# Mix matmuls cut into one piece per slot, with another order of work on VectorE and ScalarE

## The reference

```python
scores = scale * np.matmul(q, k.transpose(0, 1, 3, 2))
scores = scores + bias.transpose(2, 0, 1)[None, :, :, :]
scores = scores - np.max(scores, axis=-1, keepdims=True)
attn = np.exp(scores)
attn = attn / (np.sum(attn, axis=-1, keepdims=True) + 1e-09)
out = np.matmul(attn, v)
...
h = x @ w_in
x = (h * np.cos(h)) @ w_out
...
xn = x / rms * rms_g
g = xn @ w_gate
y = (silu(g) * (xn @ w_val)) @ w_out
```

## Time and profile before

| | |
|---|---|
| median of 3 runs | 1210.84 us |
| the profiled execution, its own time | 1210.84 us |
| its span, first to last instruction | 1209.1 us |
| busy: TensorE, weight loads | 97%, 89% |
| busy: VectorE, ScalarE, GpSimd | 58%, 41%, 40% |
| mean granted TensorE clock | 0.995 of full speed |

### The profile page before, as it was taken

How to read it: one execution, slowest core, us unless ns; L and a number is a source line. 1 busy time by engine, 2 the same in 40 slices (tenths; PEclk the granted TensorE clock), 3 DMA queues, 4 the chain that set the end, 5 groups by cost and what they waited for, 6 DMA issues and landing times. The chain is left out here.

```text
span 1209.1 us, 21829 instructions
## 1 busy us (share of the span) xinstructions
PE 1171.6 (97%) x7464; PEld 1081.3 (89%) x7464; DVE 702.2 (58%) x1540; ACT 494.7 (41%) x1034; POOL 483.8 (40%) x515
## 2 busy tenths in 40 slices
PE   5789999999989999999999999999999999999998
PEld 2268777778779999999999999999999999999998
DVE  8978888888889867777686887553011020110201
ACT  6967777777733433333343433111111111111111
POOL 3047777777776342525243353761111111111111
PEclk9989999999999999999999999999999999999999
DMA  5853525352234000000000011330000000000000
GB/s 173 248 180 119 168 93 176 100 181 75 67 108 128 19 2 1 0 0 0 0 0 0 0 35 35 105 114 27 1 1 26 0 26 0 0 26 0 26 0 26
DMA packets 46534, 69.06 MB, mean 57 GB/s; under 512 B 3712, under 2 KB 27424, under 8 KB 46496
## 3 DMA queue, kind: packets, MB, share of 16 engines
q1 hardware_dynamic: 46496, 68.60, 18.1%
HBM read 53.25 MB, written 15.34 MB: 57 GB/s over the span
## 5 line engine op out<-in xcount | busy, mean ns | idle before, releaser
L811 PE MATMUL banks<-x_high,w_low_rest 128*128 128x384 f32 x672 | 224.5, 334 | 0.0
L809 PE MATMUL banks<-x_high,w_high_rest 128*128 128x384 f32 x672 | 224.4, 334 | 0.0
L810 PE MATMUL banks<-x_low,w_high_rest 128*128 128x384 f32 x672 | 224.4, 334 | 0.0
L1358 DVE TENSOR_TENSOR X<-X,banks 128x384 f32<-128x384 f32 x72 | 39.8, 552 | 298.1 <-PE banks L811 298.0
L1377 POOL TENSOR_TENSOR product_low<-X,product_high 128x384 fp32r<-128x384 f32 x72 | 72.9, 1012 | 344.5 <-ACT product_high L1320 344.5
L1175 POOL TENSOR_TENSOR product_low<-g,product_high 128x384 fp32r<-128x384 f32 x96 | 102.6, 1069 | 236.6 <-ACT product_high L1057 236.6
L809 PE MATMUL bank<-product_high,w_high_rest 128*128 128x384 f32 x480 | 162.1, 338 | 0.8 <-POOL product_low L1175 0.8
L811 PE MATMUL bank<-product_high,w_low_rest 128*128 128x384 f32 x480 | 160.6, 335 | 0.0
L810 PE MATMUL bank<-product_low,w_high_rest 128*128 128x384 f32 x480 | 160.5, 334 | 0.0
L1085 ACT ACTIVATE angle<-angle,quarter 128x384 f32<-128x384 f32 x96 | 59.2, 617 | 202.1 <-DVE angle L1117 202.1
L588 ACT ACTIVATE probs<-probs,neg_max 128x576 f32<-128x576 f32 (+1 forms) x160 | 123.5, 772 | 18.4 <-DVE neg_max L638 18.1
(11 more groups left out here) (113 smaller groups left out, 2512.1 us busy)
## 6 DMA issues: line engine op xcount, KB each, us to landing
raw_qk<-in_qk SPq DMA_DIRECT2D x32, 576.0 KB, 3.8
bias_scratch<-bias_stage SPq DMA_DIRECT2D x36, 288.0 KB, 3.1
bias<-bias_scratch SPq DMA_DIRECT2D x32, 288.0 KB, 3.3
w_raw<-in_w_out SPq DMA_DIRECT2D x28, 256.0 KB, 2.6
values<-in_v SPq DMA_DIRECT2D x16, 320.0 KB, 4.0
w_raw<-in_w_in SPq DMA_DIRECT2D x16, 256.0 KB, 2.9
out_t<-X SPq DMA_DIRECT2D x5, 768.0 KB, 3.5
w_raw<-in_w_gate SPq DMA_DIRECT2D x12, 256.0 KB, 3.0
```

The source lines that it names most:

```text
L809: nc.tensor.matmul(out, high, x_high, start=start, stop=False)
L810: nc.tensor.matmul(out, high, x_low, start=False, stop=False)
L811: return nc.tensor.matmul(out, low, x_high, start=False, stop=stop)
```

## The change

- MIX_SLOTS is gone. `mix` takes a step c and does that step alone. Half 0 of pair n - 1 is done in slots 3 to 7 (c = 0 to 4), half 1 in slots 8 and 9 (c = 0, 1) and in slots 0 to 2 of the next pair (c = 2 to 4). Pieces c = 0 to 3 are two column matmuls; c = 4 is the full-width one. The waits stand at c = 0 and c = 4.
- EXP_LAG is 2 in place of 1: guard and invert treat the tile two slots back, normalise the one three back.
- On VectorE guard, normalise and invert stand ahead of add_bias; keep_mixed stands at the head of slot 3 (half 1) and slot 8 (half 0); keep_end comes in slot 4, in place of slot 3.
- On ScalarE the exponential of a slot stands ahead of the copy of the transposed tile.
- After pair 15 TensorE goes through ten slots without scores, so half 1's first two pieces come ahead of first_h and its other three behind it. The first of them waits for VectorE's copy of half 0.

```diff
--- before.py
+++ after.py
@@ -31,8 +31,7 @@
 TILES = 2 * NQ
 HS = S // 2
 QPAD = NQ * P
-EXP_LAG, T_LAG = 1, 4
-MIX_SLOTS = (4, 9)
+EXP_LAG, T_LAG = 2, 4
 EARLY_TILES = 3
 
 
@@ -533,22 +532,27 @@
                                                ident[0:rows, 0:rows])
                 last.then_inc(turned_ready, 1)
 
-            def mix(n, parity, half, first):
-
-                pe.wait_ge(att.values_in[parity], n * 8 + (16 - 8 * parity))
-                pe.wait_ge(copied, n * TILES + (NQ + 3) if half == 0 else (n + 1) * TILES)
-                if not (first and half == 0):
-                    pe.wait_ge(mixed_copied, n * 2 + half)
+            def mix(n, parity, half, c, first):
+
+                if c == 0:
+                    if half == 0:
+                        pe.wait_ge(att.values_in[parity], n * 8 + (16 - 8 * parity))
+
+                        pe.wait_ge(copied, n * TILES + (NQ + 3))
+                    else:
+                        pe.wait_ge(copied, (n + 1) * TILES)
+                        pe.wait_ge(last_end_copied, n + 1)
+                    if not (first and half == 0):
+                        pe.wait_ge(mixed_copied, n * 2 + half)
                 queries = slice(half * HS, (half + 1) * HS)
-                for c in range(NQ - 1):
+                if c < NQ - 1:
                     for h in range(2):
                         nc.tensor.matmul(mixed[h * D:(h + 1) * D, 0:HS], values[parity][:, c, h, :],
                                          probs_t[parity][:, h, c, queries], start=(c == 0), stop=False)
-                pe.wait_ge(end_copied, n + 1)
-                if half == 1:
-                    pe.wait_ge(last_end_copied, n + 1)
-                nc.tensor.matmul(mixed[:, 0:HS], values[parity][:, NQ - 1, :, :].rearrange("p h d -> p (h d)"),
-                                 probs_t_end[parity][:, queries], start=False, stop=True).then_inc(mixed_ready, 1)
+                else:
+                    pe.wait_ge(end_copied, n + 1)
+                    nc.tensor.matmul(mixed[:, 0:HS], values[parity][:, c, :, :].rearrange("p h d -> p (h d)"),
+                                     probs_t_end[parity][:, queries], start=False, stop=True).then_inc(mixed_ready, 1)
 
             def slot(n, parity, s, step, compute=True):
 
@@ -559,8 +563,12 @@
                         turn(n - 1, TILES - T_LAG + s, False)
                 elif compute:
                     turn(n, s - T_LAG, step == 0)
-                if step > 0 and s in MIX_SLOTS:
-                    mix(n - 1, 1 - parity, MIX_SLOTS.index(s), step == 1)
+                if s < 3:
+                    if step > 1:
+                        mix(n - 2, parity, 1, s + 2, False)
+                elif step > 0:
+                    half, c = divmod(s - 3, NQ)
+                    mix(n - 1, 1 - parity, half, c, step == 1)
 
             def pair(n, parity, step):
                 for s in range(TILES):
@@ -573,12 +581,13 @@
             with pe.Fori(1, PAIRS // 2) as m:
                 pair(m * 2, 0, 2)
                 pair(m * 2 + 1, 1, 2)
-            for s in range(MIX_SLOTS[0] + 1):
+            for s in range(TILES):
                 slot(PAIRS, 0, s, 2, compute=False)
 
             pe.wait_ge(biased, PAIRS * TILES)
             chunks.first_h(pe)
-            mix(LAST, 1, 1, False)
+            for c in range(2, NQ):
+                mix(LAST, 1, 1, c, False)
 
         @block.scalar
         def _(act):
@@ -605,11 +614,11 @@
 
             def pair(n, parity, first):
                 for s in range(TILES):
+                    exps(n, s)
                     if s >= T_LAG:
                         keep(n, parity, s - T_LAG)
                     elif not first:
                         keep(n - 1, 1 - parity, TILES - T_LAG + s)
-                    exps(n, s)
 
             pair(0, 0, True)
             pair(1, 1, False)
@@ -668,19 +677,21 @@
                     m, _, r = back(n, parity, s, EXP_LAG)
                     m3, _, r3 = back(n, parity, s, EXP_LAG + 1)
 
-                    if hp is not None:
-                        dve.wait_ge(att.bias_in[s], (hp + 1) * 16)
-                    add_bias(n, s, step == 0)
+                    if step > 1 and s == 3:
+                        keep_mixed(n - 2, 1)
+                    if step > 0 and s == 8:
+                        keep_mixed(n - 1, 0)
                     if s >= EXP_LAG or step > 0:
                         guard(m, r)
                     if (s >= EXP_LAG + 1 or step > 0) and r3 not in POOL_TILES:
                         normalise(dve, m3, r3, dve_normed)
                     if s >= EXP_LAG or step > 0:
                         invert(m, r)
-                    if step > 0 and s == T_LAG - 1:
+                    if hp is not None:
+                        dve.wait_ge(att.bias_in[s], (hp + 1) * 16)
+                    add_bias(n, s, step == 0)
+                    if step > 0 and s == 4:
                         keep_end(n - 1, 1 - parity)
-                    if step > 0 and s in MIX_SLOTS:
-                        keep_mixed(n - 1, MIX_SLOTS.index(s))
 
             pair(0, 0, 0, hp=0)
             pair(1, 1, 1)
@@ -699,6 +710,7 @@
                     normalise(dve, m3, r3, dve_normed)
                 if s < EXP_LAG:
                     invert(LAST, TILES - EXP_LAG + s)
+            keep_mixed(LAST - 1, 1)
             keep_end(LAST, 1)
             dve.wait_ge(mixed_copied, (LAST - B + 2) * 2)
             for k in DVE_PARTS:
```

## The result

The changed kernel takes 1233.3 us (median of 4 runs, 1232.49 to 1233.76), the kernel before 1210.62 us in the same comparison. The ratio is 1.0186, with a 95% interval of 1.0169 to 1.0204. The forecast was 1230, with a range of 1217 to 1240. The profiled spans are 1231.8 and 1209.1.

The account below looks back on a forecast made before the run. TensorE was taken as the bound, with about 16.0 us of work a pair. Steady pairs 15.1, pair 1 -0.7, pair 15 +3.0 and tail +1.5 sum to 18.9 on 1210.84: 1230 us, range 1217 to 1240.

Parts of the forecast that it names:

- VectorE's idle time: Steady pairs: VectorE idles 2.0 us a pair until the mix is done; better interleaving wins TensorE only 0.4 to 0.5.
- A change of form and back: TensorE going into the 64-wide form and out costs 0.34 us; a piece behind a 64-row transpose costs 0.64, not 0.83.
- The pair takes 17.66: Steady pairs 2 to 14: TensorE's work goes from 16.0 to 17.66 us, mix pieces costing 7.24 against 5.55; 15.1 in all.
- The new orders: VectorE's and ScalarE's work per pair lies under TensorE's 17.66 us, so VectorE's reordering and EXP_LAG 2 cost and win nothing.
- Part 4's tie: ScalarE's copy behind the exponential waits for its slot's addition; slot 3's transposes just covered, else up to 0.4 us, once or twice a pair.
- Pair 1 and pair 15: Pair 1 has fewer pieces and keeps 1.3 us of stalls: -0.7; the first nine slots of pair 15: +3.0.
- The tail: After pair 15, half 1's first piece waits for VectorE's copy ahead of first_h: +1.5 us, including 0.25 for a later split.

Follow-up runs that it names:

- kernel 4: Changed kernel with two-step column pieces in slots 0, 3, 5 and 8, the old tail, and ScalarE's copy ahead of its exponential: 1208.0 us.
- experiment 3: Changed kernel with each column piece as one full-width matmul in place of two of 64 columns, leaving out head 1's part of the mix: 1205.6 us.
- experiment 5: Changed kernel with EXP_LAG 1, VectorE's addition first and ScalarE's copy first, as in the kernel before: 1234.02 us.
- 6: Two-step kernel (kernel 4) with EXP_LAG 1 and VectorE's addition ahead of guard, normalise and invert: 1216.34 us.
- 9: As kernel 4, but each half's four column steps together in slot 3 or 8: 1225.66 us; also with EXP_LAG 1 and VectorE's addition first: 1238.85 us.
- experiment 7: Changed kernel with the mix in two whole blocks (slots 2, 7) and old tail: 1250.56 us; second, with ScalarE's copy ahead of its exponential: 1225.47 us.
- experiment 2: Changed kernel with 42 useless identity transposes on TensorE during the tail's wait for the copy of half 0: 1230.53 us.
- 8: Kernel before with its two whole mix blocks one slot earlier, in slots 3 and 8, and keep_end in VectorE's slot 2: 1218.72 us.
- experiment 1: Changed kernel with all five pieces of pair 15's half 1 behind first_h, as in the kernel before: 1228.53 us.

## Why the prediction was right, and where a term was off

- *TensorE is the bound, and VectorE's idle time is worth at most 0.5 a pair.* Right. VectorE's wait for the mix nearly went, and the pair grew from 16.49 to 17.70. The 0.5 was won in kernel 4, whose 16.33 are all work; its two more changes of form, which cost 0.3, leave 0.16 of it.
- *A change of form and back costs 0.34, 0.19 less behind a 64-row tile.* Right, and shown three ways: slots of 1.80, 1.90, 1.45 and 1.34 as worked out; 0.34 less per slot without the change (experiment 3); the pair at 16.33 with half the changes (experiment 4). The 0.19 is borne out by slot 8, which goes from 1.22 to 1.86, by 0.64, where slots 4 to 6 pay 0.83.
- *The pair takes 17.66.* 17.70. Over 13 pairs it is +15.7, for 15.1 forecast. The prediction's own terms (16.0 + 7.24 - 5.55) give 17.69; it wrote 17.66.
- *The new orders are hidden in the changed kernel.* Right (experiment 5). They stop being hidden when the pieces get fewer: VectorE's then wins 8 and 13 us (6 and 9), and ScalarE's costs 25 with whole blocks (7). ScalarE's order was not run with two-step pieces.
- *Part 4's tie just fits.* Right as far as it goes: no transposes wait for ScalarE in the steady pairs. Experiment 7 shows what it costs where it does not fit.
- *Pair 1 and pair 15:* -0.7 and +3.1, for -0.7 and +3.0. In pair 1 there is luck: 17.52 less 16.0 of work leaves 1.5 of stalls, not 1.65, and that 1.3 of them would stay was a guess without a row.
- *The tail:* this term was mis-sized, +1.5 forecast and +4.8 measured, and it is nearly all of the 3.3 us by which the time was missed. The wait for the copy of half 0 was seen. The copy ends 13.73 behind the last tile's score (356.91 + 0.44, and 343.62), as before (13.72); the 0.25 that was added for a later split did not come. Two things were missing.
  - The clock: TensorE's matmuls behind 4.56 us of idle time run at 1.2 GHz. The two pieces take 2.11 to the next matmul, where they take 1.12 at full clock, and each first_h matmul takes 0.32 for 0.17. Experiment 2 gives back 2.8.
  - The count of pieces: the sum has 0.63 ahead of first_h and 0.63 behind it. That is the price of one piece, but two stand in each place. At full clock they take 1.12 (357.54 to 358.66 in experiment 2, and 363.75 to 364.87 here), 1.0 more in all.

  With these, 1.5 + 2.8 + 1.0 - 0.25 is 5.05. The next stage starts 1.57 behind the last full-width piece (364.87 to 366.44), in the kernel before 1.79, which takes off 0.2 and leaves the 4.8.

By the Trainium skill (TensorE: Matmul & The Clock Gate, The HAM clock gate), the clock is gated down when TensorE has been idle; the trace agrees, with 0.50 granted from 357.50 to 363.30. The price of that belonged in the tail's term.

## What to carry to other kernels

Count how often a stream of matmuls changes the array's form (64 columns or rows against 128) before cutting a group of narrow matmuls into pieces; here each change to 64 columns and back costs 0.34 us, so pieces should be as long as the other engines allow, or stand next to a change that is there anyway, if the engine that feeds them still keeps up (it did not in 8 and 9). An idle engine beside a bound one is no loss: read the bound engine's own waits to see what the idleness costs it. The best cut was neither whole blocks nor single steps but pieces of two steps, by 0.2% over the old kernel, and the order of the engine that feeds the bound only showed its worth where pieces were few. Where a new order of work makes the bound engine idle for some microseconds (4.56 here), ask what the matmuls behind it cost at half the clock, and count the pieces there one by one.

## What the runs showed that was not expected

- The clock fell in experiment 1's tail as well, where TensorE had only gaps of under 1 us; there the pattern of work was that of the kernel before, which kept its full clock (1.00 in the tail). Of the seven kernels that have experiment 1's tail only two show it in their traces, that one and the second of experiment 7. What tips it was not settled.
- Fewer changes of form made the kernel slower when they came with uneven slots: 15.6 us of work a pair ended as 17.4. The work of the bound engine is a floor (two steps reach it, 16.33 where 16.3 was worked out). That the evenness of the slots decides how near a pair comes to it is argued from these runs; no run changed it alone.
